# Attention products in quarters of 32 array columns, six token buffers, smaller raw weight pieces and the key table first

## The chip, the cores and the metric

One core of one Trainium2 chip runs the kernel. Its time is the device time in microseconds of one execution; times of before are given as the median of three executions.

## The reference, cut to what matters

Three layers follow one another. The change touches the first, an attention with a decaying state, for 4 batches of 8 heads, 768 tokens and a head size of 48:

```python
for t in range(S):
    kt, vt, rt = (k[:, :, t], v[:, :, t], r[:, :, t])
    cur = np.einsum('bhd,bhe->bhde', u[None] * kt, vt)
    y[:, :, t] = np.einsum('bhd,bhde->bhe', rt, state + cur)
    state = w[None, :, :, None] * state + np.einsum('bhd,bhe->bhde', kt, vt)
...
logits = x @ w_gate                      # 8 experts, each takes the best 384 of 3072 tokens
h = np.maximum(x[mask] @ w1[e], 0.0); out[mask] = h @ w2[e]
...
return ((x @ w_a) * (x @ w_b)) @ w_out   # the third layer
```

## The kernel before, in words

The attention is computed in 24 tiles of 128 tokens (`NT`), six to a batch (`TPB`). Heads go in four pairs (`PAIRS`), one head on array rows 0 to 63 and one on 64 to 127 (`HALVES`). Within a tile the recurrence is turned into products: queries and keys are scaled by tables of powers of the decay (`rtab`, `ktab`), so that the score of two tokens is one dot product; a state of 48x48 a head is carried from tile to tile.

TensorE's program is written out by hand, in this order for tile n: `turn(n + 2)` transposes queries (L1057) and scaled keys (L1064) of the tile after next; `x_turn(n - 1)` transposes the finished output of the tile before (L1132); `scores(n + 1)` (L1077); `from_state(n)` (L1088), not in the first tile of a batch; `values(n)` (L1098); `update(n + 1)` (L1109), not for the last tile of a batch; `diagonals(n + 1)` (L1122), the term with `u`; `logits(n - 1)` (L1139), the routing scores. All of these are products of float32; each `pe.matmul` on float32 becomes two matmuls with a weight load each, a transpose one. Five of the six products are cut into halves of 64 array columns, so that the array works as two column tiles (`values`, `diagonals`, `logits`) or, since the two heads of a pair use different rows, as four tiles (`scores`, `from_state`); `update` writes the two heads of a pair to the two column halves.

VectorE scales queries (`scale_r`, L585), forms `rk` (L593), masks the scores (L602), adds outputs (L614) and carries the state sum (L623). ScalarE copies keys and sums out of PSUM and issues the store of the tile. GpSimd scales keys with `ktab_tok` (`scale_keys`, L429, two to three tiles ahead), multiplies the diagonal term (L438) and fades the state (L447).

SyncE's queue issues the loads. A tile's keys, queries and values are three loads of 192 KB with rows of 192 bytes, into one of four buffers (`SLOTS`); the loads of tile n + 4 wait until `values(n)` and the diagonal term of n are done. On the same queue go nine loads of 768 KB, the weights of the third layer (`load_raw`, L349, three buffers). During the attention ScalarE and GpSimd split those into an upper and a lower part, in 27 pieces of 512 columns (`upper_raw` L971, `lower_raw` L453), one or two a tile by `raw_step`.

At the start VectorE builds `decay`, `decay_rev`, then `ktab` and `rtab` together, once `w` and `u` have landed (L544 to L575). TensorE transposes `ktab` when all tables are there (`CD_TABLES`, L1144 to L1147), VectorE copies the result to `ktab_tok` (L575), and GpSimd, which waits for all of VectorE's table work (`CD_ALL`), begins with `scale_keys`.

Behind the attention comes the routing, then eight experts with the third layer (from some 210 us to the end); TensorE is busy there nearly all the time. The change leaves that part alone.

Of the kernel before, what the change touches and what calls it, by code (L numbers as in the profile page):

```python
# [11 lines left out]
P = 128  # L12
# [4 lines left out]
def attention_moe_bilinear(nc, r, k, v, w, u, w_gate, w1, w2, w_a, w_b, w_out, out, x_rows):  # L17
# [13 lines left out]
    STATES = TPB - 1  # L31
    SLOTS = 4

# [3 lines left out]
    STAGES = 3  # L37
    RAWS = DC
    PIECES = 3
    PIECE = FF // PIECES  # L40
    PARTS = 3
# [13 lines left out]
    with ctx:  # L55
# [76 lines left out]
        with ExitStack() as arena:  # L132
            def at(name, shape, dt=F32):
                return arena.enter_context(nc.sbuf_tensor(name, shape, dt))

            causal = at("causal", [P, P])
            decay = at("decay", [P, PAIRS, HALF + 1])
            decay_rev = at("decay_rev", [P, PAIRS, HALF + 1])
            w128 = at("w128", [P, PAIRS, 1])
            rtab = at("rtab", [P, PAIRS, P])  # L140
            ktab = at("ktab", [P, PAIRS, P])
            ktab_tok = at("ktab_tok", [P, PAIRS, P])
            u_col = at("u_col", [P, PAIRS, 1])
# [12 lines left out]
            state = at("state", [P, 2, PAIRS, DH])  # L156
            xs = at("xs", [P, 2, D])
            xt = at("xt", [P, DC, P])
            raw = at("raw", [P, RAWS, FF])

# [11 lines left out]

        s_w = sem("s_w")
        s_const = sem("s_const")
        s_cpool = sem("s_cpool")
        s_cdve = sem("s_cdve")
        s_cpe = sem("s_cpe")
        raw_landed = [sem(f"raw_landed{n}") for n in range(RAWS)]
        raw_hi = sem("raw_hi")
# [116 lines left out]

        OC = FF // D
        raw_chunks = [src[c * P:c * P + P, :] for src in (w_a, w_b) for c in range(DC)]
        raw_chunks += [w_out[c * OC * P:(c + 1) * OC * P, :].rearrange("(c p) d -> p c d", p=P)
                       for c in range(FFC // OC)]  # L300
        RAW_PIECES = len(raw_chunks) * PIECES
        assert len(raw_chunks) == (B - 1) * RAWS and 2 * RAWS == TPB and FFC // OC == RAWS

# [3 lines left out]
        def raw_pieces(n):  # L307

            return [(p // PIECES, p, raw[:, p // PIECES % RAWS, p % PIECES * PIECE:(p % PIECES + 1) * PIECE],
                     w_all[:, p // PIECES // RAWS, :, p // PIECES % RAWS * FF + p % PIECES * PIECE:  # L310
                           p // PIECES % RAWS * FF + (p % PIECES + 1) * PIECE])
                    for p in range(RAW_PIECES) if raw_step(p) == n]

        HALVES = [slice(0, HALF), slice(HALF, P)]

        def updates(n):
# [15 lines left out]
        def _(sp):  # L332
# [10 lines left out]

            def load_raw(c):

                s = c % RAWS
                if c >= RAWS:
                    sp.wait_ge(raw_lo, (c - RAWS + 1) * PIECES)
                sp.dma_start(raw[:, s, :] if c < (B - 2) * RAWS else raw[:, s, :].rearrange("p (c d) -> p c d", d=D),  # L349
                             raw_chunks[c]).then_inc(raw_landed[s], 16)  # L350

            sp.wait_ge(s_cpool, 3)
            for n in range(SLOTS):
                load(n)
# [12 lines left out]

        @block.gpsimd
        def _(pool):
# [49 lines left out]
            assert made[0] == CP_ALL + 1  # L419

            pool.wait_ge(s_cdve, CD_ALL)

# [27 lines left out]
            def lower_raw(n):  # L450
                for c, p, piece, cols in raw_pieces(n):
                    pool.wait_ge(raw_hi, p + 1)
# [83 lines left out]
        def _(dve):  # L536
# [6 lines left out]

            dve.wait_ge(s_w, 64)  # L544
            dve.memset(decay_rev[:, :, HALF:HALF + 1], 1.0)
# [9 lines left out]

            dve.reciprocal(ktab[:, :, HALF:HALF + QUARTER], decay[:, :, 1:QUARTER + 1])
            step(dve.reciprocal(rtab[:, :, HALF - QUARTER:HALF], decay_rev[:, :, HALF - QUARTER:HALF]))
            n = QUARTER
            while n < HALF:
                dve.tensor_tensor(ktab[:, :, HALF + n:HALF + 2 * n], ktab[:, :, HALF:HALF + n],  # L560
                                  ktab[:, :, HALF + n - 1:HALF + n].to_broadcast([P, PAIRS, n]), ALU.mult)
# [3 lines left out]
            dve.tensor_copy(ktab[:, :, 0:HALF], decay_rev[:, :, 1:HALF + 1])  # L565
            step(dve.tensor_copy(rtab[:, :, HALF:P], decay[:, :, 0:HALF]))
# [358 lines left out]
        def _(act):  # L925

            act.wait_ge(s_cpool, 2)
            for h2 in range(2):
                rows = slice(h2 * HALF, h2 * HALF + DH)
                act.dma_start(decay[rows, :, 1:2], w[h2:H:2, :].rearrange("a (d o) -> d a o", o=1),  # L930
                             allow_slow_non_contiguous=True).then_inc(s_w, 16)
                act.dma_start(u_col[rows, :, :], u[h2:H:2, :].rearrange("a (d o) -> d a o", o=1),
                             allow_slow_non_contiguous=True).then_inc(s_w, 16)

# [33 lines left out]
            def upper_raw(n):  # L968
                for c, p, piece, cols in raw_pieces(n):
                    act.wait_ge(raw_landed[c % RAWS], 16 * (c // RAWS + 1))  # L970
# [79 lines left out]
        def _(pe):  # L1050
# [17 lines left out]
            def scores(n):  # L1068
# [12 lines left out]
            def from_state(n):  # L1081
# [3 lines left out]
                for a in range(PAIRS):  # L1085
                    for h2 in range(2):
                        for ih in HALVES:
                            pe.matmul(pY[h2][ih, a, :], rs[HALVES[h2], n % 3, a, ih], state[HALVES[h2], n % 2, a, :],  # L1088
                                      start=(a == 0), stop=False, skip_group_check=True)

            def values(n):
                if n >= 1:
                    pe.wait_ge(x_ready, n)
                for h2 in range(2):
                    pe.wait_ge(am_ready, 2 * n + h2 + 1)
                    for a in range(PAIRS):
                        for ih in HALVES:
                            last = pe.matmul(pY[h2][ih, a, :], am[:, n % 2, h2, a, ih], vt[:, n % SLOTS, 2 * a + h2, :],  # L1098
# [4 lines left out]
            def update(n):  # L1103
# [3 lines left out]
                for a in range(PAIRS):  # L1107
                    for h2 in range(2):
                        last = pe.matmul(pU[HALVES[h2], a, :], ktok[:, n % 3, 2 * a + h2, :],  # L1109
                                         vt[:, n % SLOTS, 2 * a + h2, :], start=True, stop=True)  # L1110
                last.then_inc(update_done, 1)

            def diagonals(n):

                pe.wait_ge(rk_ready, n + 1)
                if n >= 1:
                    pe.wait_ge(dsum_ready, n)
                if n >= 2:
                    pe.wait_ge(xt_ready, n - 1)
                for a in range(PAIRS):  # L1120
                    for ih in HALVES:
                        last = pe.matmul(pD[ih, :], rk[:, n % 2, a, ih], uw[:, a * H:a * H + H],  # L1122
# [12 lines left out]
            def logits(n):  # L1135
                pe.wait_ge(xt_ready, n + 1)
                for c in range(DC):
                    for ih in HALVES:
                        last = pe.matmul(pL[ih, :], xt[:, c, ih], gate_w[:, c, :], start=(c == 0), stop=(c == DC - 1),  # L1139
# [222 lines left out]

CD_TABLES, CD_ALL = 11, 14
CHAIN = 69
# [25 lines left out]
```

## Time and profile before

| | before |
|---|---|
| median of 3 runs | 907.1 us (906.6 to 907.97) |
| profiled execution: time, span | 912.4 us, 910.7 us |
| TensorE matmuls: busy, count | 839.8 us (92%), 7941 |
| VectorE, ScalarE, GpSimd busy | 534.4, 234.7, 423.5 us |
| mean granted TensorE clock | 0.957 |
| attention stage, 0 to 165 us: matmuls | 3436 |

The span is cut into windows and groups; a busy share alone does not tell what ends a stage. A matmul group's length in the timeline runs from the first start to the last modelled end; where groups follow one another, the distance between their starts is the better measure of their cost. "issue" is time in which the engine waited for nothing that the profile shows.

### The profile page before, as it was taken

Reading aid. Unit: us, or ns where it says so; the run is one execution under the profiler, and the core shown is the slowest. Engines: PE = TensorE matmul, PEld = TensorE weight load, DVE = VectorE, ACT = ScalarE, POOL = GpSimd, SP = SyncE. Lnnn points to the kernel's source line nnn. Section 1 sums busy time; section 2 is a strip of 40 time slices with the busy share of each in tenths; the row PEclk is TensorE's granted clock in tenths of the full one; section 3 lists DMA queues with packets and bytes.
Section 4 is the critical chain, followed back from the end, with each engine's and each line's share of the span. In section 5 each row is a group of like instructions: output and inputs, shape, how many; then the busy total and the mean of one; then the engine's idle time right before and its main releaser. Section 6 shows DMA issues by size and latency. Waiting matters only on the chain.

```text
span 910.7 us, 19299 instructions
## 1 busy us (share of the span) xinstructions
PE 839.8 (92%) x7941; PEld 805.3 (88%) x7941; DVE 534.4 (59%) x1295; ACT 234.7 (26%) x502; POOL 423.5 (47%) x457
## 2 busy tenths in 40 slices
PE   4989989419999999999999999999999999999995
PEld 3878879318899999999999999999999999999994
DVE  4665556576767676667667765767577422631321
ACT  1333222012222223312331232213222322231221
POOL 4565657057127704760575067317631770475001
PEclk9998889657999999999999999999999999999998
DMA  9596763023012101210121012012111210121000
GB/s 209 128 224 146 192 156 91 19 71 95 1 35 87 53 18 48 84 62 1 64 76 53 13 68 79 35 36 69 53 36 36 79 53 27 58 80 55 1 1 27
DMA packets 93112, 61.82 MB, mean 68 GB/s; under 512 B 79200, under 2 KB 83808, under 8 KB 93024
## 3 DMA queue, kind: packets, MB, share of 16 engines
q0 software_dynamic: 11008, 34.61, 11.7%
q1 hardware_dynamic: 77728, 21.25, 11.1%
q10 hardware_dynamic: 4288, 4.72, 1.5%
q8 instruction: 63, 1.03, 0.4%
q14 instruction: 25, 0.20, 0.1%
HBM read 51.13 MB, written 9.44 MB: 67 GB/s over the span
## 4 chain that ended last, share of the span: by engine, by line
PE 76%; DVE 3%; issue 1%; POOL 1%; DMA 1%; ACT 0%; ACTq 0%; POOLq 0%; DVEq 0%
PE bank L1239 40%; PE bank L1313 16%; PE bank L1282 10%; PE bank L1295 2%; PE bank L1262 2%; DVE mask_mem L676 1%; PE bank L1299 1%; PE bank L1179 1%; PE bank L1230 1%; PE bank L1195 1%; DMA wst<-in_moe_w,rows_i 1%; PE bank L1187 1%; PE bank L1220 0%; DVE cand L672 0%; POOL w L499 0%
## 5 line engine op out<-in xcount | busy, mean ns | idle before, releaser
L1239 PE MATMUL bank<-act,w_all 128*128 128x384 f32 x1584 | 295.9, 338 | 0.0
L1239 PEld LDWEIGHTS bank<-act,w_all 128*128 128x128 f32 x1584 | 275.3, 188 | 0.0
L1313 PE MATMUL bank<-w_all,gs 128*128 128x384 f32 x864 | 167.4, 337 | 0.3 <-DVE gs L869 0.3
L482 POOL DMA_INDIRECT wst<-in_moe_w,rows_i x48 | 52.3, 1090 | 245.4 <-DVE rows_i L746 192.4
L499 POOL TENSOR_TENSOR w<-wst,w 128x384 fp32r<-128x384 f32 (+1 forms) x106 | 130.3, 1229 | 43.9 <-ACT w L1005 38.2
L1313 PEld LDWEIGHTS bank<-w_all,gs 128*128 128x128 f32 x864 | 150.0, 188 | 0.6 <-DVE gs L869 0.6
L1282 PE MATMUL bank<-hs,w 128*128 128x384 f32 x576 | 113.0, 340 | 0.0
L866 DVE TENSOR_TENSOR ga<-ga,bank 128x384 f32<-128x384 f32 x96 | 53.0, 552 | 86.1 <-PE bank L1239 77.4
L1282 PEld LDWEIGHTS bank<-hs,w 128*128 128x128 f32 x576 | 100.5, 188 | 0.0
L1239 PE MATMUL bank<-act,w 128*128 128x384 f32 x504 | 99.6, 341 | 0.0
L1026 ACT ACTIVATE gs<-ga 128x384 fp32r<-128x384 f32 x96 | 50.5, 526 | 188.8 <-DVE ga L866 188.8
L869 DVE TENSOR_TENSOR gs<-ga,gs 128x384 fp32r<-128x384 f32 x96 | 60.2, 627 | 56.8 <-ACT gs L1026 53.9
L1239 PEld LDWEIGHTS bank<-act,w 128*128 128x128 f32 x504 | 88.8, 190 | 0.0
L486 POOL DMA_INDIRECT wst<-in_moe_w,rows_i x64 | 63.8, 996 | 51.0 <-POOL w L499 35.0
L844 DVE SCALAR_TENSOR_TENSOR hs<-bank,hs 128x384 fp32r<-128x384 f32 x64 | 35.6, 556 | 80.7 <-ACT hs L1010 78.2
L1023 ACT ACTIVATE ga<-bank 128x384 f32<-128x384 f32 x96 | 47.1, 490 | 126.7 <-PE bank L1239 94.0
L1010 ACT ACTIVATE hs<-bank 128x384 fp32r<-128x384 f32 x64 | 31.5, 492 | 162.1 <-PE bank L1239 135.7
L524 POOL DMA_INDIRECT out<-os_,ids_now x24 | 23.9, 995 | 69.2 <-ACT os_ L1036 63.2
L429 POOL TENSOR_TENSOR ktok<-kt,ktab_tok 128x384 f32<-128x384 f32 x24 | 23.9, 1000 | 44.5 <-DMA vt<-in_v 37.9
L1005 ACT ACTIVATE w<-wst 128x512 fp32r<-128x512 f32 (+1 forms) x50 | 30.3, 619 | 47.6 <-DMA wst<-in_moe_w,rows_i 47.3
L676 DVE TENSOR_TENSOR mask_mem<-key_hi,cand 128x480 f16<-128x480 f32 x42 | 37.4, 930 | 0.7
L602 DVE TENSOR_TENSOR am<-bank,causal 128x512 f32<-128x512 f32 x48 | 30.8, 682 | 7.8 <-PE bank L1077 7.7
(179 smaller groups left out, 1047.5 us busy)
## 6 DMA issues: line engine op xcount, KB each, us to landing
kt<-in_k SPq DMA_DIRECT2D x24, 192.0 KB, 3.1
rt<-in_r SPq DMA_DIRECT2D x24, 192.0 KB, 4.3
vt<-in_v SPq DMA_DIRECT2D x24, 192.0 KB, 4.5
x_rows<-xs ACTq DMA_DIRECT2D x24, 192.0 KB, 3.2
raw<-in_moe_w_a SPq DMA_DIRECT2D x3, 768.0 KB, 6.5
raw<-in_moe_w_b SPq DMA_DIRECT2D x3, 768.0 KB, 5.6
raw<-in_moe_w_out SPq DMA_DIRECT2D x3, 768.0 KB, 6.4
wst<-in_moe_w,rows_i POOLq DMA_INDIRECT x112
```

Source lines behind the costliest of these rows:

```text
L482: pool.indirect_dma_start(wst[:, k % STAGES, :], None, w1_rows, bass.IndirectOffsetOnAxis(ap=rows_i[:, k:k + 1], axis=0)).then_inc(wst_lan ...
L486: pool.indirect_dma_start(wst[:, k % STAGES, 0:D], None, w2_rows, bass.IndirectOffsetOnAxis(ap=rows_i[:, k:k + 1], axis=0)).then_inc(wst_l ...
L499: pool.tensor_tensor(lo, src, hi.bitcast(F32), ALU.subtract).then_inc(w_split, 1)
L676: dve.tensor_tensor(mask[:, js, :], keys[:, js].rearrange("p (j o) -> p j o", o=1).to_broadcast([P, NT // 2, CAND]), cand[:, :].rearrange( ...
L844: dve.scalar_tensor_tensor(hs2[:, f % 2, 1, :], ring[f % 2][:, 0:CAP], 0.0, hs2[:, f % 2, 0, :].bitcast(F32), ALU.max, ALU.subtract).then_ ...
L866: dve.tensor_tensor(ga[:, c % 2, :], ga[:, c % 2, :], ring[2 * (c % 2) + 1][:, 0:CAP], ALU.mult).then_inc(g_ready, 1)
L869: dve.tensor_tensor(gs2[:, c % 2, 1, :], ga[:, c % 2, :], gs2[:, c % 2, 0, :].bitcast(F32), ALU.subtract).then_inc(gs_lo, 1)
L1023: act.activation(ga[:, c % 2, :], ring[2 * (c % 2)][:, 0:CAP], ACT.Copy).then_inc(as_ready, 1)
L1026: act.activation(gs2[:, c % 2, 0, :], ga[:, c % 2, :], ACT.Copy).then_inc(gs_hi, 1)
L1239: last = pe.matmul(dst, wt(a), mv(b), start=(n == 0 and (a, b) == (0, 0)), stop=(n == len(pairs) - 1 and (a, b) == (1, 0)))
L1282: last = pe.matmul(acc[c][:, 0:CAP], w2_2[:, a, f, c * P:c * P + P], hs2[:, f % 2, b, :], start=(f == 0 and (a, b) == (0, 0)), stop=(f == ...
L1313: last = pe.matmul(acc[t][:, 0:D], gs2[:, c % 2, a, t * P:t * P + P], wo2[:, b, c, :], start=(c == 0 and (a, b) == (0, 0)), stop=(c == FFC ...
```

## The change

The six products take quarters of 32 array columns; `update` slices a pair's 128 columns in quarters, so that each half-used head of 64 becomes two. `SLOTS` goes from 4 to 6. The raw weights come in 18 pieces of 768 columns, each its own load of 384 KB, in three buffers. `ktab` is completed before `rtab`, the transposes wait for it alone (`CD_KEYS`), ScalarE copies the result, and a semaphore `table_ready` tells GpSimd and the first `diagonals` of it. `w` and `u` have semaphores of their own.

```diff
-    SLOTS = 4
+    SLOTS = 6
...
-    RAWS = DC
-    PIECES = 3
-    PIECE = FF // PIECES
+    RAWS = 3
+    PIECE = 2 * D
+    SPAN = DC * FF
...
-            raw = at("raw", [P, RAWS, FF])
+            raw = at("raw", [P, RAWS, PIECE])
...
+        QUARTERS = [slice(q * P // 4, (q + 1) * P // 4) for q in range(4)]
...
-            def load_raw(c):
-
-                s = c % RAWS
-                if c >= RAWS:
-                    sp.wait_ge(raw_lo, (c - RAWS + 1) * PIECES)
-                sp.dma_start(raw[:, s, :] if c < (B - 2) * RAWS else raw[:, s, :].rearrange("p (c d) -> p c d", d=D),
-                             raw_chunks[c]).then_inc(raw_landed[s], 16)
+            def load_raw(p):
+
+                if p >= RAWS:
+                    sp.wait_ge(raw_lo, p - RAWS + 1)
+                piece = raw[:, p % RAWS, :]
+                if p * PIECE >= (B - 2) * SPAN:
+                    piece = piece.rearrange("p (c d) -> p c d", d=D)
+                sp.dma_start(piece, raw_sources[p]).then_inc(raw_landed[p % RAWS], 16)
...
-                if n == 0:
+                if n == 1:
                     sp.dma_start(gate_w[:, :, :], w_gate.rearrange("(c p) e -> p c e", p=P)).then_inc(s_const, 16)
-            for c in range(RAWS):
-                load_raw(c)
+                if n >= SLOTS - RAWS:
+                    load_raw(n - SLOTS + RAWS)
...
-                for c in range(RAWS, len(raw_chunks)):
-                    if raw_step((c - RAWS + 1) * PIECES - 1) + 1 == n:
-                        load_raw(c)
+                for p in range(RAWS, RAW_PIECES):
+                    if raw_step(p - RAWS) + 1 == n:
+                        load_raw(p)
...
+            pool.wait_ge(table_ready, 1)
             pool.wait_ge(s_cdve, CD_ALL)
...
-            dve.wait_ge(s_w, 64)
+            dve.wait_ge(s_w, 32)
...
             dve.wait_ge(s_cpool, CP_IDENT + 2)
+            dve.wait_ge(s_u, 32)
...
-            dve.wait_ge(s_cpe, 1)
-            step(dve.tensor_copy(ktab_tok[:, :, :], bank[7][:, :].rearrange("p (a t) -> p a t", a=PAIRS)))
...
+            act.wait_ge(s_cpe, 1)
+            act.activation(ktab_tok[:, :, :], bank[7][:, :].rearrange("p (a t) -> p a t", a=PAIRS), ACT.Copy
+                           ).then_inc(table_ready, 1)
...
-                        for jh in HALVES:
+                        for jh in QUARTERS:
                             last = pe.matmul(pA[h2][jh, a, :], ks[HALVES[h2], n % 2, a, jh],
...
-                        for ih in HALVES:
+                        for ih in QUARTERS:
                             pe.matmul(pY[h2][ih, a, :], rs[HALVES[h2], n % 3, a, ih], state[HALVES[h2], n % 2, a, :],
...
-                        for ih in HALVES:
+                        for ih in QUARTERS:
                             last = pe.matmul(pY[h2][ih, a, :], am[:, n % 2, h2, a, ih], vt[:, n % SLOTS, 2 * a + h2, :],
...
-                    for h2 in range(2):
-                        last = pe.matmul(pU[HALVES[h2], a, :], ktok[:, n % 3, 2 * a + h2, :],
-                                         vt[:, n % SLOTS, 2 * a + h2, :], start=True, stop=True)
+                    pair = ktok[:, n % 3, 2 * a:2 * a + 2, :].rearrange("p h d -> p (h d)")
+                    for q, dq in enumerate(QUARTERS):
+                        last = pe.matmul(pU[dq, a, :], pair[:, dq], vt[:, n % SLOTS, 2 * a + q // 2, :],
+                                         start=True, stop=True)
...
+                if n == 0:
+                    pe.wait_ge(table_ready, 1)
...
-            pe.wait_ge(s_cdve, CD_TABLES)
+            pe.wait_ge(s_cdve, CD_KEYS)
```

`diagonals` and `logits` take `QUARTERS` in the same way.

## Rows read from the trace of the kernel before

**Rows 1.** The page: engines over the span (busy, share, xinstructions), and the queue of instructions.

```profile
span 910.7 us, 19299 instructions
PE 839.8 (92%) x7941; PEld 805.3 (88%) x7941; DVE 534.4 (59%) x1295; ACT 234.7 (26%) x502; POOL 423.5 (47%) x457
...
q8 instruction: 63, 1.03, 0.4%
```

**Rows 2.** Windows, whole attention stage: length, busy (x) by engine, clock, DMA share, GB/s.

```profile
20.00:165.00 145.00, 131.63 (x3376) 121.14 (x3372) 85.93 (x160) 43.25 (x121) 88.11 (x92) 0.92 0.65 156
```

**Rows 3.** Timeline of TensorE's matmuls, one undisturbed tile: start, length, line, operands, count.

```profile
106.89 0.66 PE L1057 MATMUL bank<-ident,rt 128*128 128x128 f32 x4
...
108.24 1.10 PE L1077 MATMUL bank<-rs,ks 64*64 64x128 f32 x32
109.16 0.63 PE L1088 MATMUL bank<-state,rs 64*64 64x48 f32 x32
109.72 1.14 PE L1098 MATMUL bank<-vt,am 128*64 128x48 f32 x32
110.69 0.64 PE L1109 MATMUL bank<-vt,ktok 128*64 128x48 f32 x16
111.16 0.60 PE L1122 MATMUL bank<-uw,rk 128*64 128x8 f32 x16
111.61 0.50 PE L1139 MATMUL bank<-gate_w,xt 128*64 128x8 f32 x12
112.04 0.33 PE L1057 MATMUL bank<-ident,rt 128*128 128x128 f32 x1
```

**Rows 4.** Timeline of the weight loads in the same tile.

```profile
109.72 1.01 PEld L1098 LDWEIGHTS bank<-vt,am 128*64 128x64 f32 x32
...
111.11 0.55 PEld L1122 LDWEIGHTS bank<-uw,rk 128*64 128x64 f32 x16
```

**Rows 5.** Timeline of TensorE's matmuls: first row behind each stall, idle time in brackets.

```profile
51.87 0.33 PE L1088 MATMUL bank<-state,rs 64*64 64x48 f32 x8 [0.46 <-issue]
...
117.92 0.22 PE L1122 MATMUL bank<-uw,rk 128*64 128x8 f32 x1 [1.01 <-issue]
...
124.52 0.46 PE L1122 MATMUL bank<-uw,rk 128*64 128x8 f32 x11 [0.43 <-issue]
...
131.19 0.38 PE L1098 MATMUL bank<-vt,am 128*64 128x48 f32 x6 [2.01 <-issue]
```

**Rows 6.** Windows between stalls of TensorE (x in brackets: matmuls, then weight loads).

```profile
35.50:51.50 16.00, 15.20 (x375) 14.00 (x374) 9.22 (x15) 5.85 (x16) 11.74 (x12) 0.89 0.78 187
51.50:78.70 27.20, 24.36 (x626) 22.15 (x626) 17.18 (x33) 7.59 (x21) 17.82 (x18) 0.94 0.73 177
78.70:117.40 38.70, 35.74 (x875) 33.04 (x875) 22.76 (x42) 11.71 (x32) 24.16 (x26) 0.87 0.73 173
```

**Rows 7.** DMA view, windows at 49.2-49.4, 52.95-53.05, 122.1-122.3, 128.7-128.9, 132.4-132.5 us: packets starting.

```profile
q8 instruction: 1, 0.02, 27.5%
...
q8 instruction: 1, 0.02, 73.2%
...
q8 instruction: 1, 0.02, 31.1%
...
q8 instruction: 1, 0.02, 36.6%
...
q8 instruction: 1, 0.02, 69.5%
```

**Rows 8.** Windows of one microsecond inside the last of those stalls.

```profile
130.00:131.00 1.00, 0.00 (x0) 0.00 (x0) 0.00 (x0) 0.00 (x0) 1.00 (x2) 1.00 0.00 0
```

**Rows 9.** DMA view of the attention stage, 20 to 165 us: queue of instructions.

```profile
q8 instruction: 27, 0.44, 1.3%
```

**Rows 10.** TensorE's waits, 17 to 165 us: who for whom, total, times, longest.

```profile
PE bank L1057 <- DMA vt<-in_v: 2.9, 2, 1.6
```

**Rows 11.** Timeline of the start: VectorE's copy of the key table.

```profile
12.71 0.69 DVE L575 COPY ktab_tok<-bank 128x512 f32<-128x512 f32 x1 [0.77 <-PE bank L1146]
```

More of the change, by code:

```diff
@@ L173, in attention_moe_bilinear @@
         s_w = sem("s_w")
+        s_u = sem("s_u")
         s_const = sem("s_const")
@@ L177, in attention_moe_bilinear @@
         s_cpe = sem("s_cpe")
+        table_ready = sem("table_ready")
         raw_landed = [sem(f"raw_landed{n}") for n in range(RAWS)]
@@ L294, in attention_moe_bilinear @@
         w2_rows = w2.rearrange("e f d -> (e f) d")
[L297 to L302, printed above, removed]
+        raw_sources = [src[c * P:c * P + P, o:o + PIECE] for src in (w_a, w_b) for c in range(DC)
+                       for o in range(0, FF, PIECE)]
+        raw_sources += [w_out[c * P:(c + PIECE // D) * P, :].rearrange("(c p) d -> p c d", p=P)
+                        for c in range(0, FFC, PIECE // D)]
+        RAW_PIECES = len(raw_sources)
+        assert RAW_PIECES * PIECE == (B - 1) * SPAN
         def raw_step(p):
@@ L307, in raw_pieces @@
         def raw_pieces(n):
-            return [(p // PIECES, p, raw[:, p // PIECES % RAWS, p % PIECES * PIECE:(p % PIECES + 1) * PIECE],
-                     w_all[:, p // PIECES // RAWS, :, p // PIECES % RAWS * FF + p % PIECES * PIECE:
-                           p // PIECES % RAWS * FF + (p % PIECES + 1) * PIECE])
+            return [(p, raw[:, p % RAWS, :],
+                     w_all[:, p * PIECE // SPAN, :, p * PIECE % SPAN:p * PIECE % SPAN + PIECE])
                     for p in range(RAW_PIECES) if raw_step(p) == n]
         HALVES = [slice(0, HALF), slice(HALF, P)]
+        QUARTERS = [slice(q * P // 4, (q + 1) * P // 4) for q in range(4)]
         def updates(n):
@@ L450, in lower_raw @@
             def lower_raw(n):
-                for c, p, piece, cols in raw_pieces(n):
+                for p, piece, cols in raw_pieces(n):
                     pool.wait_ge(raw_hi, p + 1)
@@ L553, in _ @@
                 n *= 2
-            dve.reciprocal(ktab[:, :, HALF:HALF + QUARTER], decay[:, :, 1:QUARTER + 1])
+            dve.tensor_copy(ktab[:, :, 0:HALF], decay_rev[:, :, 1:HALF + 1])
+            step(dve.reciprocal(ktab[:, :, HALF:HALF + QUARTER], decay[:, :, 1:QUARTER + 1]))
+            n = QUARTER
+            while n < HALF:
+                step(dve.tensor_tensor(ktab[:, :, HALF + n:HALF + 2 * n], ktab[:, :, HALF:HALF + n],
+                                       ktab[:, :, HALF + n - 1:HALF + n].to_broadcast([P, PAIRS, n]), ALU.mult))
+                n *= 2
+            assert made[0] == CD_KEYS
+            dve.tensor_copy(rtab[:, :, HALF:P], decay[:, :, 0:HALF])
             step(dve.reciprocal(rtab[:, :, HALF - QUARTER:HALF], decay_rev[:, :, HALF - QUARTER:HALF]))
@@ L559, in _ @@
             while n < HALF:
-                dve.tensor_tensor(ktab[:, :, HALF + n:HALF + 2 * n], ktab[:, :, HALF:HALF + n],
-                                  ktab[:, :, HALF + n - 1:HALF + n].to_broadcast([P, PAIRS, n]), ALU.mult)
                 step(dve.tensor_tensor(rtab[:, :, HALF - 2 * n:HALF - n], rtab[:, :, HALF - n:HALF],
@@ L564, in _ @@
                 n *= 2
-            dve.tensor_copy(ktab[:, :, 0:HALF], decay_rev[:, :, 1:HALF + 1])
-            step(dve.tensor_copy(rtab[:, :, HALF:P], decay[:, :, 0:HALF]))
             step(dve.tensor_tensor(w128[:, :, :], decay[:, :, HALF:HALF + 1], decay[:, :, HALF:HALF + 1], ALU.mult))
             dve.wait_ge(s_cpool, CP_IDENT + 2)
+            dve.wait_ge(s_u, 32)
             for h2 in range(2):
@@ L931, in _ @@
                              allow_slow_non_contiguous=True).then_inc(s_w, 16)
+            for h2 in range(2):
+                rows = slice(h2 * HALF, h2 * HALF + DH)
                 act.dma_start(u_col[rows, :, :], u[h2:H:2, :].rearrange("a (d o) -> d a o", o=1),
-                             allow_slow_non_contiguous=True).then_inc(s_w, 16)
+                             allow_slow_non_contiguous=True).then_inc(s_u, 16)
             def copy_keys(n):
@@ L968, in upper_raw @@
             def upper_raw(n):
-                for c, p, piece, cols in raw_pieces(n):
-                    act.wait_ge(raw_landed[c % RAWS], 16 * (c // RAWS + 1))
+                for p, piece, cols in raw_pieces(n):
+                    act.wait_ge(raw_landed[p % RAWS], 16 * (p // RAWS + 1))
                     act.activation(cols[:, 0, :], piece, ACT.Copy).then_inc(raw_hi, 1)
+            act.wait_ge(s_cpe, 1)
+            act.activation(ktab_tok[:, :, :], bank[7][:, :].rearrange("p (a t) -> p a t", a=PAIRS), ACT.Copy
+                           ).then_inc(table_ready, 1)
             copy_keys(0)
@@ L1120, in diagonals @@
                 for a in range(PAIRS):
-                    for ih in HALVES:
+                    for ih in QUARTERS:
                         last = pe.matmul(pD[ih, :], rk[:, n % 2, a, ih], uw[:, a * H:a * H + H],
@@ L1137, in logits @@
                 for c in range(DC):
-                    for ih in HALVES:
+                    for ih in QUARTERS:
                         last = pe.matmul(pL[ih, :], xt[:, c, ih], gate_w[:, c, :], start=(c == 0), stop=(c == DC - 1),
@@ L1359, in _ @@
             expert(E - 1, False, False)
-CD_TABLES, CD_ALL = 11, 14
+CD_KEYS, CD_ALL = 10, 15
 CHAIN = 69
```

## The prediction

> **What bounds the kernel now.** I read the page first: TensorE is busy 92% of the span, over 7941 matmuls each with a weight load [rows 1], so the question is what TensorE does where the change works. The windows by stage say where that is: the attention stage, up to 165 us of the 911, holds 3376 of those matmuls at a mean granted clock of 0.92; VectorE works 85.9 us there, GpSimd 88.1, and the DMA engines are 65% busy [rows 2]. That is 3.6, 3.7 and 3.9 us for each of the 24 token tiles. TensorE's own timeline of one undisturbed tile shows 5.16 us from one `turn` to the next (106.89 to 112.04) with its groups back to back [rows 3]. So an undisturbed tile is bound by TensorE, and the stage, at some 6 us a tile, is longer than that by its disturbances.
>
> What paces a group comes from its start-to-start times. `values` (48 columns moved) takes 0.97 us for 16 steps of two column tiles, `diagonals` (8 columns) 0.45 us for 8 such steps [rows 3]; the loads alone span 1.01 us for 32 and 0.55 us for 16 [rows 4]. That is some 58 ns a step for both, though the columns moved differ sixfold. So the weight load of 64 columns paces these, not the matmul. `scores` moves 128 columns in 8 steps of four tiles, 0.92 us to the next group's first matmul, 0.11 us a step: there the matmul paces.
>
> Then the disturbances. In six places, four of them shown, the trace has TensorE idle in the middle of a group, between two matmuls with the same operands and no wait between them; what released it is given as "issue" [rows 5]. Between those places the windows count matmuls and loads: 375 + 374, then 626 + 626, then 875 + 875 (the middle windows end at two more such stalls) [rows 6]. These are 3, 5 and 7 times 250. The page's queue of kind "instruction" moved 1.03 MB in 63 packets, 16 KB each, over the span, for 15,882 loads and matmuls, 252 a packet [rows 1]. So TensorE's instructions come in blocks of one packet each, a little over 250 matmuls and loads with a few waits among them, and TensorE stops where a block ends and the next has not landed. The windows of the DMA view time the packets: they start at 49.3, 122.2 and 128.8 us, and TensorE resumes at 51.87, 124.52 and 131.19, that is 2.3 to 2.6 us behind each start [rows 5, 7]. While it stood still, from 130 to 131 us, the DMA engines moved nothing [rows 8]: this is latency, not bandwidth. The fetch after a block was entered starts 1.1 us later at 51.87, 1.2 us at 131.19, but 4.3 us at 117.92 and 4.3 us at 124.52, where the token and raw weight loads keep the DMA engines at work. If blocks were fetched several ahead, no stall could end just behind the start of a fetch. I take it that one block is fetched while one is executed. A block then takes at least 1.2 + 2.4 = 3.6 us, and 6.6 to 6.7 us in the two cases with traffic (117.92 to 124.52 to 131.19). Today a block holds over 4 us of TensorE's work, so most fetches just fit.
>
> **The change, part by part.** *Quarters.* Each of the six products issues twice as many matmuls, each with its own load, of half the array columns. For `scores`, `values` and `diagonals` that is 32, 32 and 16 more a tile in 24 tiles, `logits` 12 more in 24, `from_state` 32 and `update` 16 more (there the two `h2` products become four) in 20 tiles: 768 + 768 + 384 + 288 + 640 + 320 = 3168 matmuls, and 6336 instructions with their loads. At 250 to 256 a block that is 25 more blocks. What it can give back: the load-paced steps hold four tiles instead of two with half the columns each. If loads of the column tiles run side by side and their time goes with the columns, a step falls from 58 ns to about 29, or to the 41 ns that 48 moved columns take by the pace of `scores` (0.11 us for 128): `values` 16 x 17 ns, `update` 8 x 17, `diagonals` 8 x 29, `logits` 6 x 29, and some 0.1 us in `from_state`, 0.9 us a tile; `scores` stays. The other bound is nothing, if the array's 128 columns are loaded at one rate whatever their split. I take the gain as likely but it does not set the time, for the reason that follows: a tile then has 291 pairs instead of 151, 2.3 blocks, to be executed in 4.3 us, 1.9 us a block, against a fetch of 3.6 us or more.
>
> *The sum.* 27 blocks were fetched between 20 and 165 us [rows 9]; with the 25 it is 52. The first two blocks stand ready at the start (63 packets cover all but the head of the program) and the first fetch lands near 24.5 us, as now. Some 50 blocks follow, each at the pace of its fetch. The floor is 3.6 us. To it comes the wait behind loads: 3.9 us of DMA work a tile [rows 2] in a tile of some 10 us is a share of 0.4, and a fetch that meets such a burst waits half of it, 2 us: 0.8 us in the mean, 4.4 us a block; the last six tiles, whose loads are over, keep 3.6. Mean 4.25. The stage then ends near 24.5 + 50 x 4.25 = 237 us instead of 165: 72 us later. Bounds: 3.6 us for all gives 204.5 us (+40); 5.0 us, between the floor and the 6.6 us seen, gives 274.5 (+110). I take 4.25, nearer the floor, since in longer tiles the DMA engines are idle more of the time. TensorE idle half the time may well lose its full clock; at 1.2 GHz a block's 1.9 us become 3.8, still within such a fetch.
>
> The Trainium skill's page "Runtime: NRT & Kernel Launch", section "Instruction fetch mechanics", says that instructions come in 16 KiB blocks of 256, two of them held, and that the fetch is hidden since a sequencer needs some 20 cycles an instruction. The block agrees with the 252 a packet; the hiding doesn't: `from_state`'s 32 pairs run in 0.63 us [rows 3], 10 ns an instruction. By the page 582 instructions would themselves take about as long as the fetches, and no fetch would be seen.
>
> *Six buffers.* Loads are issued two tiles sooner. It removes what TensorE waits for a load: 2.9 us in two waits [rows 10], and the low clock behind them, 2 to 4 us. In a stage paced by fetches that is covered: 0. It moves nothing ahead of the start: 6 x 576 + 3 x 384 KB in front, as before 4 x 576 + 3 x 768. *Raw pieces.* 18 pieces of 768 columns instead of 27 of 512: the same columns through ScalarE and GpSimd, one GpSimd subtraction about 1.9 us instead of 1.3; with 40% idle there, 0 (0.6 us a tile, if that cover is gone). *Key table.* The transposes no longer wait for `rtab`'s half of the table work, nor for `u`; the copy of the table goes from VectorE, 0.69 us at 12.71 [rows 11], to ScalarE. The first keys come up to 1.3 us earlier, or no earlier, since GpSimd still waits for all of VectorE's tables; -1 us. Waits added: GpSimd's first `scale_keys` and TensorE's first `diagonals` on the new semaphore, both behind a copy of 0.7 us; nobody else is queued there.
>
> Sum: 907.1 + 72 - 1 = 978. The profiled execution took 912.4 us with a span of 910.7, 0.6% over the median; the parts are durations that differ by as little, so I add them to the median.
>
> **The rivals.** (a) *Fetches stay hidden and the loads gain* (faster). If more than one block is held ahead, the six stalls are something else and quarters cost nothing: 24 x 0.9 = 22 us less, with 4 us of load stalls gone and half of that given back to waits on ScalarE and VectorE; the tile, 4.3 us, stays over the 3.9 us of DMA work. Time 886, decided by a block's fetch being under 1.9 us. For it: most of the 27 fetches cause no stall today. Against: the fetch was never under 2.3 us, and stalls stand on block ends. (b) *No change*: column tiles share the load's time and fetches stay hidden: 905. For it: nothing in the trace has 32 columns. Against: the same evidence as (a). (c) *An issue floor per pair* (slower, another cause). The Trainium skill's page "TensorE: Matmul & The Clock Gate", section "Back-to-back issue gap", has a floor of 25 ns between matmuls. By it 291 pairs would take 7.3 us a tile, 51 us more in all. As a mechanism of this kernel, if the 29 ns a pair of `scores` and `values` (32 in 0.92 and 0.97 us) were the sequencer's pace: 291 x 29 ns are 8.4 us a tile, 3.3 over 5.16, 78 us in all: 984. Against it stands `from_state` with 0.56 us for 32, 17.5 ns a pair [rows 3]; for it, only that this is a short burst. Told apart by the gaps, not by the time.
>
> **How the numbers follow.** Forecast (fetch-bound) 0.80, centre 978; (a) 0.10, (b) 0.05, (c) 0.05. The range holds the forecast's bounds, less their last ends, and (c): 938 to 1015. Slower 0.85, same 0.05, faster 0.10; 0.2% (1.8 us) is about what a measurement can tell.
>
> **What would show it.** Right: about 88 packets in the instruction queue; 11,100 matmuls; TensorE with a gap of 1 to 3 us at "issue" about every 250 matmuls and loads, twice or more in each tile; the attention stage ending at 205 to 275 us; the share of DMA work below 0.5 there; the stages behind it unchanged. The load gain would show inside a block as `diagonals` in about half its 0.45 us. Wrong: gaps no more frequent than today (then (a) or (b), told apart by that same group), or steps of one even pace of 25 ns with no gaps (c). Were the load bursts harmless to fetches, the stage would end near 205 us; were each fetch behind a burst, beyond 275.

## The result, and the profile after

| | before | after |
|---|---|---|
| median | 907.5 us (4 runs, 906.6 to 909.9) | 986.3 us (4 runs, 983.6 to 989.1) |
| ratio | | 1.086 (95% interval 1.084 to 1.089) |
| profiled execution: time, span | 912.4, 910.7 us | 989.1, 987.0 us |
| last product of the attention | 164.7 us | 239.2 us |
| packets in the instruction queue | 63 | 88 |
| mean granted clock | 0.957 | 0.919 |

The change makes the kernel 79 us slower by the medians; 978 was forecast. Between the two profiled executions the spans differ by 76.3 us, and nearly all of it lies in the attention stage: it ends 74.5 us later, and what follows is about as long as it was (746 and 748 us). The page of after, with the rows that answer to [rows 1]:

```profile
span 987.0 us, 25624 instructions
PE 857.5 (87%) x11109; PEld 816.1 (83%) x11109; DVE 543.8 (55%) x1294; ACT 235.7 (24%) x494; POOL 422.7 (43%) x448
...
PEclk9778777795569999999999999999999999999998
...
q8 instruction: 88, 1.44, 0.6%
```

11,109 matmuls are 3168 more than before, to the one counted out ahead, and 88 packets are 25 more. TensorE's mean clock is under 0.9 in eight of the ten slices that hold the attention. The window over that stage, 20 us to its last product, after (columns as in [rows 2]):

```profile
20.00:239.20 219.20, 147.04 (x6376) 130.03 (x6364) 94.86 (x155) 42.40 (x109) 83.38 (x80) 0.77 0.46 108
```

The instruction packets in the same stretch, from the DMA view:

```profile
q8 instruction: 51, 0.84, 1.7%
```

Of 219.2 us TensorE is busy 147.0, idle 72.2; before it was some 131 of 145, so idle 13 to 14 [rows 2]. Idle time takes some 59 of the 74.5 us, and the busy time, which should have fallen, rises by 15.6 (before, up to 164.7 us, it was 131.4). The clock says why: a mean of 0.77, where the trace's two levels are full and half (2.4 and 1.2 GHz), is half the clock for 46% of the stage, 101 us; before it was 0.92, some 23 us. What the low level costs shows in one group, `scores`, in windows of after: with the clock at 0.50 its 64 matmuls take 1.70 us to the next group, at 1.00 they take 0.90 (34.36 to 35.26 in the timeline below).

```profile
26.30:28.00 1.70, 1.70 (x65) 1.68 (x72) 0.69 (x1) 1.31 (x3) 0.10 (x1) 0.50 0.99 238
34.30:35.30 1.00, 1.00 (x71) 0.94 (x74) 0.56 (x2) 1.00 (x3) 1.00 (x3) 1.00 1.10 220
```

51 fetches in 219.2 us is one in 4.3 us.

The idle time stands where the forecast put it. TensorE's waits of after, 17 to 240 us (total, times, longest):

```profile
PE bank L1154 <- issue: 17.1, 8, 2.4
PE bank L1137 <- issue: 15.3, 7, 2.6
PE bank L1100 <- issue: 12.2, 10, 2.9
PE bank L1110 <- issue: 11.8, 8, 3.2
PE bank L1089 <- issue: 8.2, 6, 2.8
PE bank L1122 <- issue: 5.1, 3, 1.9
PE bank L1147 <- ACT logit L975: 2.2, 3, 1.1
PE bank L1076 <- issue: 1.4, 2, 1.2
```

That is 71 us at "issue" in 44 gaps, where before there were six. If all of TensorE's records in the trace are counted, its semaphore instructions among them, the 44 gaps stand whole multiples of 256 apart, and so do the six of before. The wait for a token load [rows 10] is gone. Two stretches of TensorE's timeline of after:

```profile
28.03 0.90 PE L1100 MATMUL bank<-state,rs 64*32 64x48 f32 x64
28.86 0.89 PE L1110 MATMUL bank<-vt,am 128*32 128x48 f32 x64
29.57 0.52 PE L1122 MATMUL bank<-vt,ktok 128*32 128x48 f32 x32
29.91 0.30 PE L1137 MATMUL bank<-uw,rk 128*32 128x8 f32 x16
32.56 0.28 PE L1137 MATMUL bank<-uw,rk 128*32 128x8 f32 x13 [2.36 <-issue]
...
34.36 1.16 PE L1089 MATMUL bank<-rs,ks 64*32 64x128 f32 x64
35.26 0.29 PE L1100 MATMUL bank<-state,rs 64*32 64x48 f32 x11
36.90 0.71 PE L1100 MATMUL bank<-state,rs 64*32 64x48 f32 x53 [1.35 <-issue]
37.54 0.89 PE L1110 MATMUL bank<-vt,am 128*32 128x48 f32 x64
```

The matmuls and loads between these stalls and the next one, in windows of after:

```profile
32.30:36.70 4.40, 2.99 (x126) 2.66 (x125) 2.56 (x3) 1.96 (x5) 3.20 (x4) 1.00 0.74 143
36.70:40.00 3.30, 1.68 (x127) 1.48 (x128) 1.43 (x4) 0.00 (x0) 1.30 (x1) 1.00 0.09 18
```

`diagonals` stops in the middle, its fetch having started in the window 29.7 to 29.9 us (below), and goes on at 32.56, 2.7 us later; the next two blocks hold 251 and 255 matmuls and loads [rows 6]. In the second of them TensorE works 1.68 us of 3.30, at full clock, with the DMA engines nearly idle (0.09), ScalarE idle and GpSimd busy for 1.30 us. So neither a lack of DMA bandwidth nor a busy neighbour explains that gap. The window of the DMA view at 29.7 to 29.9 us:

```profile
q1 hardware_dynamic: 118, 0.02, 75.1%
q8 instruction: 1, 0.02, 41.6%
```

Inside a block the quarters do what they are for. `values` takes 0.71 us to the next group (28.86 to 29.57) against 0.97 [rows 3]. For `diagonals`, which a stall cuts in that tile, the timeline of a later one:

```profile
57.27 0.89 PE L1110 MATMUL bank<-vt,am 128*32 128x48 f32 x64
57.97 0.44 PE L1137 MATMUL bank<-uw,rk 128*32 128x8 f32 x31
58.25 0.19 PE L1154 MATMUL bank<-gate_w,xt 128*32 128x8 f32 x1
```

`diagonals`, from 57.97 to 58.25, is 0.28 us against 0.45 [rows 3].

### The profile page after: what moved, and what is told of

The parts are those of the page before. It is cut to its first block, busy times and chain, and to the rows that moved or that the text cites. A ratio compares the mean times of both kernels' runs of the same rounds, so it can differ in the third digit from the quotient of the medians.

```text
span 987.0 us, 25624 instructions
## 1 busy us (share of the span) xinstructions
PE 857.5 (87%) x11109; PEld 816.1 (83%) x11109; DVE 543.8 (55%) x1294; ACT 235.7 (24%) x494; POOL 422.7 (43%) x448
## 4 chain that ended last, share of the span: by engine, by line
PE 85%; issue 9%; DVE 3%; POOL 1%; DMA 1%; ACT 0%; ACTq 0%; POOLq 0%; DVEq 0%
PE bank L1254 37%; PE bank L1328 15%; PE bank L1297 10%; PE bank L1089 4%; PE bank L1110 3%; PE bank L1069 2%; PE bank L1076 2%; PE bank L1100 2%; PE bank L1310 2%; PE bank L1277 2%; PE bank L1147 1%; PE bank L1137 1%; PE bank L1122 1%; DVE mask_mem L683 1%; PE bank L1314 1%
## 5 line engine op out<-in xcount | busy, mean ns | idle before, releaser
L442 POOL TENSOR_TENSOR dv<-vt,dsum 128x384 f32<-128x384 f32 x24 | 19.9, 831 | 130.2 <-ACT dsum L958 130.2
L1089 PE MATMUL bank<-rs,ks 64*32 64x128 f32 x1536 | 40.0, 345 | 8.2 <-issue 8.2
L600 DVE TENSOR_TENSOR rk<-rs,ks 128x512 f32<-128x512 f32 x24 | 33.7, 1403 | 19.0 <-ACT ks L950 18.9
```

## The experiments

Each kernel was timed beside the kernel before on the same chip; ratios are to it.

**Quarters alone.** The kernel before with the quarters of the six products and nothing else.

```diff
-                        for jh in HALVES:
+                        for jh in QUARTERS:
...
-                        for ih in HALVES:
+                        for ih in QUARTERS:
...
+                    pair = ktok[:, n % 3, 2 * a:2 * a + 2, :].rearrange("p h d -> p (h d)")
+                    for q, dq in enumerate(QUARTERS):
+                        last = pe.matmul(pU[dq, a, :], pair[:, dq], vt[:, n % SLOTS, 2 * a + q // 2, :],
+                                         start=True, stop=True)
```

> The kernel before with the quarters alone: four buffers, large raw pieces and the old order of the tables stay. Theory (the stage goes at the pace of instruction fetches, and the quarters double the instructions): 88 packets in the instruction queue, stage end later by 78 us and more, 985 to 995 us; a little slower than the whole change, since its tables are done some 4 us later and TensorE waits for loads again. Rival (buffers or raw pieces have a part in the loss): under 970 us.

Measured: 987.1 us, ratio 1.089 (1.084 to 1.095), 88 packets. The whole loss is in the quarters.

The trace of this run shows something more. Its first fetch starts at 22.2 us, that of the changed kernel at 17.1, 5 us sooner; both kernels then fetch 52 blocks up to the end of the stage, and the stages end within 1 us of each other (TensorE's last product at 238.6 and 239.2 us). So a block takes 4.24 us here and 4.35 in the changed kernel, fetch to fetch, and the earlier start is lost on the way. Why its blocks are slower no run isolates.

**The rest alone.** The changed kernel with halves again: six buffers, smaller pieces, key table first.

```diff
-                        for jh in QUARTERS:
+                        for jh in HALVES:
...
-                    for q, dq in enumerate(QUARTERS):
+                    for h2 in range(2):
```

> The changed kernel with halves again: six buffers, smaller raw pieces and the key table first stay. Theory: 63 packets, the start is some 4 us earlier than before, the two load waits of 2.9 us and the low clock behind them are gone: 896 to 902 us. Rival (those parts cost in the changed kernel): 907 us or more.

Measured: 901.1 us, ratio 0.993 (0.991 to 0.996), 63 packets. The other parts are a gain of 6.6 us. Together with quarters they give nothing: 986.3 and 987.1 us are the same. The six buffers have no wait left to remove there: the quarters alone show no wait for a token load even with four. The earlier start is not covered by the fetches, since they too begin 5 us sooner; it is lost to the longer blocks named above.

**Scores with whole columns.** The kernel of "the rest alone", with half the instructions in the scores.

```diff
-                        for jh in HALVES:
-                            last = pe.matmul(pA[h2][jh, a, :], ks[HALVES[h2], n % 2, a, jh],
-                                             rs[HALVES[h2], n % 3, a, :], start=True, stop=True)
+                        last = pe.matmul(pA[h2][:, a, :], ks[HALVES[h2], n % 2, a, :],
+                                         rs[HALVES[h2], n % 3, a, :], start=True, stop=True)
```

> As e2_rest_alone, but the scores take all 128 array columns: half the matmuls and loads there, 16 fewer of each a tile, 3 blocks fewer in all. Theory: the scores are paced by the 128 columns moved, so their length stays at 0.9 us a tile; fewer stalls at block ends: 2 to 5 us under e2_rest_alone. Rival (two tiles in the place of four cost array time): a group of scores of up to 1.8 us and a time some 20 us over e2_rest_alone.

Measured: 892.9 us, ratio 0.985 (0.981 to 0.988), 60 packets: the fastest kernel of this study, 15 us under the one before. It is 8.2 us under "the rest alone", more than the 2 to 5 us that were expected. An undisturbed tile of it (121.31 to 126.68) takes 5.37 us, longer than the 5.16 of [rows 3]:

```profile
121.31 0.66 PE L1069 MATMUL bank<-ident,rt 128*128 128x128 f32 x4
...
122.66 1.16 PE L1088 MATMUL bank<-rs,ks 64*128 64x128 f32 x16
123.75 0.68 PE L1099 MATMUL bank<-state,rs 64*64 64x48 f32 x32
...
126.68 0.66 PE L1069 MATMUL bank<-ident,rt 128*128 128x128 f32 x4
```

The scores cost 1.09 us to the next group instead of 0.92, where they were expected to stay at 0.9, and the kernel is faster all the same: its attention stage (windows 20 to 142.6 us) has TensorE busy 118.15 of 122.60 us at a clock of 1.00, and its waits at "issue" come to one. The windows of "the rest alone" and of this kernel, and then two of this kernel's waits:

```profile
20.00:151.30 131.30, 118.67 (x3278) 110.20 (x3273) 87.73 (x155) 41.31 (x109) 87.81 (x80) 0.99 0.74 177
20.00:142.60 122.60, 118.15 (x2895) 108.54 (x2893) 84.22 (x151) 41.19 (x109) 86.93 (x80) 1.00 0.83 189
```

```profile
PE bank L1145 <- ACT logit L975: 3.4, 4, 1.1
...
PE bank L1152 <- issue: 0.4, 1, 0.4
```

TensorE's busy time is the same in both (118.7 and 118.2 us) and so, nearly, is the clock. The 8.7 us between the two windows are idle time, and the gaps at "issue" account for nearly all of it: 8.6 us in 11 gaps of "the rest alone", 0.4 us in one here.

**The same edit in the kernel before.**

> The kernel before with one edit: the scores take all 128 array columns, half the matmuls and loads there, 3 blocks fewer. Theory: the group's length stays near 0.9 us and stalls at block ends become rarer, as e3_scores_whole against e2_rest_alone (8 us): 898 to 903 us. Rival (the gain there hung on the six buffers): 905 us or more.

Measured: 903.8 us, ratio 0.996 (0.994 to 0.998). The direction holds, the size is half that beside six buffers; the expected 898 to 903 was just missed. Its trace has the gaps at "issue" down from 5.8 us to 0.3, as beside six buffers, but TensorE's waits for token loads and for scaled keys are up from 3.9 us to 7.1: with four buffers a part of the gain goes back to those.

**No token loads behind the first six tiles.** The changed kernel; later tiles read the buffers as they are, so the loads and the tokens' values are left out of the computation.

```diff
-                    load(n + SLOTS)
+                    for _ in range(3):
+                        sp.sem_inc(in_landed[(n + SLOTS) % SLOTS], 16)
```

> The changed kernel without the token loads from tile 6 on (old data are used again; output not the reference's); raw weight loads and stores stay. Theory (a fetch waits behind bursts of loads): blocks at 3.6 to 3.8 us instead of 4.35 from 35 us on, stage shorter by 25 to 35 us, 950 to 960 us. Rival (the fetch's length doesn't depend on loads): 980 us or more.

Measured: 965.8 us in a single execution, above the expected 950 to 960 and far from the rival's 980. The attention stage ends at 217.3 us, 22 earlier; window and instruction packets over 20 to 217.3 us:

```profile
20.00:217.30 197.30, 132.64 (x6347) 118.26 (x6338) 91.14 (x155) 42.18 (x109) 85.11 (x80) 0.87 0.24 66
```

```profile
q8 instruction: 51, 0.84, 1.8%
```

51 fetches in 197.3 us are one in 3.87 us instead of 4.30. The wait behind loads is there, and its share of the loss is about 21 of 79 us (986.3 less 965.8); some 58 us stay with a DMA share of 0.24. The mean without token loads is higher than 3.6 us, and the clock still at 0.87.

The traces show where the loads act. In the changed kernel TensorE goes on 2.57 us after the start of the fetch it stands for, and the next fetch starts 1.83 us after that (means of its 44 gaps); without token loads the two are 2.43 and 1.56 us (41 gaps). Both parts shrink, by 0.41 us together, and that is the difference of 4.30 and 3.87. These are one trace each.

**No-ops.** Halves, with four instructions that do nothing behind each product.

```diff
+                for _ in range(4):
+                    pe.nop(nofuse=True)
```

> As e2_rest_alone (halves), with four instructions that do nothing behind each of the 70 products of a tile: about as many instructions as with quarters, 6700 more, 26 blocks, but the array's work of the halves. Theory (the count of instructions alone costs): stalls at block ends as in the changed kernel, blocks 4.0 to 4.4 us apart, 975 to 1000 us. Rival (the loss lies in 32-column tiles, not in the count): 901 us plus what the no-ops take by themselves, seen as a longer group without idle time at block ends.

Measured: 905.1 us in a single execution, but with 63 packets, as many as without them: the no-ops did not come into the program. The run decides nothing; it is one more measurement of "the rest alone", 4 us over that one's median and 1 us over its slowest.

**The same count in three shapes.** In place of the no-ops, three kernels with 64 more matmuls and loads a tile than "the rest alone", 69 packets each. The first has quarters in `values`, where the array gains; the second has no 32-column tile and moves the columns of the scores in two halves; the third has quarters in the scores.

```diff
-                        for ih in HALVES:
+                        for ih in QUARTERS:
                             last = pe.matmul(pY[h2][ih, a, :], am[:, n % 2, h2, a, ih], vt[:, n % SLOTS, 2 * a + h2, :],
```

> As e2_rest_alone, quarters in the values product alone: 64 instructions more a tile, 6 blocks more, 6.5 us of array time less in all by the 0.69 against 0.97 us of that group. Theory: a block is used up in about 3.4 us, under the 4.3 us of a fetch, so the saving is lost and the 33 blocks set the stage: 905 to 912 us. Rival (it pays as long as only one product is split): 893 to 897 us.

```diff
-                    for h2 in range(2):
-                        for jh in HALVES:
-                            last = pe.matmul(pA[h2][jh, a, :], ks[HALVES[h2], n % 2, a, jh],
-                                             rs[HALVES[h2], n % 3, a, :], start=True, stop=True)
+                    for ts in HALVES:
+                        for h2 in range(2):
+                            for jh in HALVES:
+                                last = pe.matmul(pA[h2][jh, a, ts], ks[HALVES[h2], n % 2, a, jh],
+                                                 rs[HALVES[h2], n % 3, a, ts], start=True, stop=True)
```

> As e2_rest_alone, but each product of the scores is issued twice, for 64 moved columns each, the stationary part unchanged at 64 array columns: 64 instructions more a tile, 6 blocks more, no 32-column tile anywhere. The array's work stays about the same (two steps of 58 ns, paced by the load, for one of 109). Theory (the count of instructions costs, whatever their shape): 69 packets, 915 to 925 us, as e6_quarters_in_values, which has the same count. Rival (32-column tiles are what costs): 901 to 906 us.

```diff
-                        for jh in HALVES:
+                        for jh in QUARTERS:
                             last = pe.matmul(pA[h2][jh, a, :], ks[HALVES[h2], n % 2, a, jh],
```

> As e2_rest_alone, quarters in the scores alone: again 64 instructions more a tile, 6 blocks, array work as before (paced by 128 moved columns). Theory: 915 to 925 us, within 5 us of e9_scores_two_moving_halves. Rival (tile shape): 10 us and more over e9.

Measured: 920.1 us (ratio 1.015, 1.011 to 1.020), 921.1 us (1.013, 1.008 to 1.019) and 923.3 us (1.014, 1.009 to 1.019). The scores' groups of the second and the third are equally long:

```profile
100.18 1.16 PE L1090 MATMUL bank<-rs,ks 64*64 64x64 f32 x64
```

```profile
103.30 1.16 PE L1089 MATMUL bank<-rs,ks 64*32 64x128 f32 x64
```

Six blocks more cost 19 to 22 us over the 901.1 us of "the rest alone", with 32-column tiles or without, and even where the array's work falls. So the count costs, not the shape. The second and third came out as expected (915 to 925 us, within 5 us of each other). The first expectation, 905 to 912 us, was too low: it took the slower of two paces where both vary from block to block.

**Near the threshold.** The kernel with whole scores, quarters in `diagonals` (first), and in `logits` as well (second).

```diff
-                    for ih in HALVES:
+                    for ih in QUARTERS:
                         last = pe.matmul(pD[ih, :], rk[:, n % 2, a, ih], uw[:, a * H:a * H + H],
```

> As e3_scores_whole, quarters in the diagonals: as many instructions as e2_rest_alone (302 a tile), 0.2 us a tile less in the diagonals. Theory: 4.2 us of work a block, just at the pace of a fetch: the gain of up to 4.5 us is about used up by more stalls, 890 to 894 us. Rival (fetches stay hidden): 888 us.

> As e7, logits in quarters too: 326 instructions a tile, 3.8 us of work a block, under a fetch's pace. Theory: slower than e7 by 3 to 8 us although the array works 0.15 us a tile less. Rival: 3 us faster than e7.

Measured: 902.3 us (ratio 0.994, 0.992 to 0.997) and 906.4 us (0.998, 0.996 to 0.999), 63 and 65 packets. The first is 9.4 us slower than whole scores alone, where at most 1 was expected, though the array works less: again the count is what the time follows. Its trace has 6.8 us of gaps at "issue" in 8 places where whole scores alone had 0.4 us in one, and a clock of 0.97 where that one had 1.00. The second is 4.1 us slower than the first, within the expected 3 to 8.

**Quarters with whole scores.** The changed kernel with the scores' edit.

> The changed kernel (quarters in five products), but the scores take all 128 array columns: 96 instructions a tile less than the changed kernel, 9 blocks less (43 instead of 52 in the attention stage). Theory (the stage is its blocks times 4.35 us): 39 us less than the changed kernel, 945 to 955 us. Rival (the pace is set by something that goes with tiles of tokens, not with blocks): 975 us or more.

Measured: 958.5 us (ratio 1.054, 1.048 to 1.059), 79 packets. 28 us less for nine blocks, 3.1 us a block, not 4.35, and above the expected 945 to 955. Its window and packets, 20 us to its last product:

```profile
20.00:207.50 187.50, 137.18 (x5233) 121.38 (x5232) 90.62 (x151) 42.28 (x109) 84.42 (x80) 0.83 0.54 125
```

```profile
q8 instruction: 42, 0.69, 1.6%
```

That is a fetch in 4.46 us, slower than the changed kernel's 4.30: with fewer instructions a block holds more of the array's work.

All kernels with the full computation, by matmuls and loads in a tile with all six products:

| matmuls and loads a tile | kernel | packets | median us |
|---|---|---|---|
| 270 | whole scores, six buffers | 60 | 892.9 |
| 302 | the rest alone | 63 | 901.1 |
| 302 | whole scores, quarters in diagonals | 63 | 902.3 |
| 326 | and in logits | 65 | 906.4 |
| 366 | quarters in values | 69 | 920.1 |
| 366 | scores in two moving halves | 69 | 921.1 |
| 366 | quarters in scores | 69 | 923.3 |
| 486 | changed kernel, whole scores | 79 | 958.5 |
| 582 | changed kernel | 88 | 986.3 |

The first and the last differ by 28 packets and 93.4 us, 3.3 us a packet, and equal counts give equal times within 3.3 us.

## Why the prediction was right

*The mechanism.* Fetches of blocks set the pace of the stage. Its marks came out: 88 packets, 11,109 matmuls, gaps at "issue" in the midst of groups, blocks of a little over 250 matmuls and loads, the DMA share 0.46 where below 0.5 was said, the later stages unchanged. That the count of instructions causes it is shown by the three kernels of equal count; that loads lengthen the fetches is shown by the kernel without them. That one block is fetched ahead, and not more, is read from the traces; no run changes it. They are clear on it: in each of the 44 gaps of after TensorE goes on 2.2 to 3.4 us after the start of the latest fetch, and in all 52 blocks of its stage the next fetch starts only 0.8 to 3.4 us after TensorE's first record of the block.

*The sum.* A block in 4.25 us was forecast, the trace has 4.30; a stage end at 237 us, the trace has 239.2. That closeness is partly luck, since several terms were off and cancelled. The sum's own terms, 4.4 us for 18 tiles and 3.6 for six, have a mean of 4.2 and not 4.25, which would end the stage at 234.5 us. The first fetched block was taken to land near 24.5 us, as before; after, its fetch starts at 17.1 us and TensorE goes on with it at 19.5, 5 us sooner. The floor of 3.6 us was too low as a mean: without token loads a block takes 3.87 us, raw loads and stores still running. The wait behind loads, put at 0.8 us a block for 18 tiles and so 0.6 in the mean, is 0.43 (4.30 less 3.87). The floor was taken from the two shortest fetches, where the fetches of a whole stage, and blocks whose own work exceeds a fetch, make the mean.

*The clock.* "At 1.2 GHz a block's 1.9 us become 3.8, still within such a fetch" was right about the level and too light about the price. The stage ran at 1.2 GHz for 46% of its length. Windows of after show one such turn: full clock up to 41.8 us with TensorE busy 8.28 of 13.60 us, then half the clock with 8.60 busy of 10.20, and full clock again from 52.0 us.

```profile
28.20:41.80 13.60, 8.28 (x522) 7.58 (x507) 6.57 (x13) 2.20 (x7) 4.76 (x5) 1.00 0.68 144
41.80:52.00 10.20, 8.60 (x292) 7.46 (x290) 4.17 (x7) 2.06 (x5) 4.78 (x5) 0.50 0.39 92
```

Work of 3.8 us against a fetch of 3.6 to 4.3 does not hide in every block. Without token loads the stage became 22 us shorter at a clock of 0.87. By the windows 14.4 of those 22 us are busy time of TensorE (147.04 to 132.64) and 7.5 idle, while the fetches' own two parts, above, account for some 21 us (0.41 us in 51 blocks). Both readings hold together if the fetches set the length and a lower clock fills time that would have been idle; that is my reading, and no run holds the clock fixed to test it.

*The load gain*, taken as likely: confirmed inside the blocks (`diagonals` 0.28 for 0.45 us, `values` 0.71 for 0.97). Rival (b) had the column tiles share the load's time, so that nothing is gained; these groups refute it, and fit loads of different column tiles that run side by side and shorten with their columns. The guess of 41 ns for a step of `values` is met (0.71 us for 16 steps, 44 ns). `from_state` was to gain 0.1 us and lost some 0.2: 53 of its matmuls take 0.64 us at full clock (36.90 to 37.54), so 64 some 0.77, where 32 had taken 0.56 [rows 3]. That is 12 ns a pair of matmul and load, and the 64 of `values` take 11; whether the two stand at one pace that no split can go under, no run tells.

*Other terms.* "Key table, -1 us": the table's transposes started 4.0 us sooner, and no longer wait for `rtab`. TensorE's timelines of before and of after:

```profile
11.52 1.09 PE L1146 MATMUL bank<-ident,ktab 128*128 128x128 f32 x4 [11.52 <-DVE rtab L566]
```

```profile
7.49 1.09 PE L1161 MATMUL bank<-ident,ktab 128*128 128x128 f32 x4 [7.49 <-DVE ktab L564]
```

With halves the three side parts gain 6.6 us; in the changed kernel 0.8 us, inside the noise. "In a stage paced by fetches that is covered: 0" agrees with the runs for the buffers. The key table was mis-sized and its gain did not arrive: the forecast of up to 1.3 us was 4.0 us at the transposes and 5 us at the first fetch, and a stage of fetches that begins sooner should end sooner. Against the quarters alone it does not, because its blocks are 0.11 us longer (4.35 and 4.24 us); what in the other parts makes them so stays open.

*The rivals.* (a) fell by its own condition, a fetch under 1.9 us. Its time was added up wrongly: 907.1 less 22, less 4, with 2 given back, is 883 and not 886. (b) fell with its reason. The range's lower end, 938, has no term under it either: 3.6 us for all blocks gives 946. (c), a pace of 29 ns a pair, came nearest in time, 984 us, and is refuted by the timeline: 12 ns a pair, and the lost time stands in gaps. The Trainium skill's issue floor of about 25 ns ("TensorE: Matmul & The Clock Gate", section "Back-to-back issue gap") does not hold for these matmuls in tiles of the array, which follow one another every 11 to 12 ns. The Trainium skill also says that fetches are hidden by the pace of issue ("Runtime: NRT & Kernel Launch", section "Instruction fetch mechanics"). That does not hold here: a block ran in 1.68 us of TensorE's work, less than the 2.2 to 3.4 us from the start of a fetch to TensorE going on, and the 71 us at "issue" are fetches that were not hidden.

## What to carry to other kernels

Count a stage's TensorE instructions against its time: where 256 of them hold less than some 4 to 5 us of work here ("the rest alone", at 4.6 us a fetch, still lost 8.6 us to gaps, whole scores, at 5.1 us, 0.4), the fetch of the next block begins to set the pace, and splitting a product for the array's sake loses more than it gains. The page shows it beforehand: gaps at "issue" in the midst of a group, matmuls and loads between two such gaps in multiples of about 250. A split that doesn't shorten its group (here the scores, paced by the columns moved) should be undone, even at a small cost in array time.

## What the runs showed of the hardware that was not expected

The price does not begin at the point where the mean work of a block falls under the mean fetch. From 270 to 302 matmuls and loads a tile, where a block still holds over 4 us of work, three more packets already cost 8 to 9 us, and the kernel with 270 has one gap at "issue" of 0.4 us left against 11 gaps with 8.6 us. Both the fetch and the work of a block vary: two stalls of the changed kernel that follow each other are 2.36 and 1.35 us long. My reading, which no run isolates, is that each long fetch that meets a short block is lost. The clock comes on top only further on: it is 0.99 with 302 matmuls and loads a tile ("the rest alone"), 0.77 with 582. And an edit that makes an undisturbed tile 0.2 us longer made the kernel 8 us faster: 5.16 us a tile was never what the stage ran at.
